# A recurrence in pairs of groups with two MLPs: another order of the work at the end and the start of a pair

## The reference

```python
batch, n_heads, seq, head_dim = (4, 8, 768, 40)
for t in range(S):                       # state: one 40x40 matrix for each of 32 heads
    y[:, :, t] = np.einsum('bhd,bhde->bhe', rt, state)
    Sa = np.einsum('bhde,bhe->bhd', state, at)
    state_decay = state * wt[:, :, None, :] - np.einsum('bhd,bhe->bhde', Sa, bt)
    state = state_decay + np.einsum('bhd,bhe->bhde', vt, kt)
# y as tokens: x (3072, 320)
h = x @ w_in; g = h - np.tanh(h); x = g @ w_out          # d_ff 2048
p = domain_probs / (domain_probs.sum(-1, keepdims=True) + 1e-09)
for e in range(4):                                        # F 1024
    out += p[:, e:e + 1] * (np.maximum(x @ w1[e], 0.0) @ w2[e])
```

## Time and profile before

| | us |
|---|---|
| median of three runs | 1610.46 (1609.79 to 1610.70) |
| the profiled execution, its own time | 1605.92 |
| its span, first to last instruction | 1604.2 |
| PE busy | 1459.2 (91%) |
| DVE busy | 834.7 (52%) |
| ACT busy | 397.8 (25%) |
| POOL busy | 364.9 (23%) |

### The profile page before, as it was taken

How to read it: one execution, slowest core, us unless ns; L and a number is a source line. 1 busy time by engine, 2 the same in 40 slices (tenths; PEclk the granted TensorE clock), 3 DMA queues, 4 the chain that set the end, 5 groups by cost and what they waited for, 6 DMA issues and landing times.

```text
span 1604.2 us, 37826 instructions
## 1 busy us (share of the span) xinstructions
PE 1459.2 (91%) x15888; PEld 1276.4 (80%) x15888; DVE 834.7 (52%) x1460; ACT 397.8 (25%) x814; POOL 364.9 (23%) x310
## 2 busy tenths in 40 slices
PE   2287687999999999999969999999999999999998
PEld 1266566977987887887858888999999999999898
DVE  7978765967967876854213233333333333333333
ACT  1022342333233333333324222111111111111111
POOL 4121453323334332321324301001020202020000
PEclk9988798999999999999989999999999999999999
DMA  7554584056047136121030220101010101000011
GB/s 186 146 138 118 155 204 128 21 142 178 25 121 186 37 95 152 29 65 38 5 106 1 86 70 1 36 0 36 0 36 0 36 0 36 0 0 0 0 49 49
DMA packets 87672, 108.72 MB, mean 68 GB/s; under 512 B 13630, under 2 KB 66686, under 8 KB 87542
## 3 DMA queue, kind: packets, MB, share of 16 engines
q1 hardware_dynamic: 87542, 106.83, 24.8%
HBM read 75.94 MB, written 30.84 MB: 67 GB/s over the span
## 4 chain that ended last, share of the span: by engine, by line
PE 79%; issue 7%; DVE 6%; POOL 3%; POOLq 2%; DMA 1%; ACT 1%; SPq 1%; DVEq 0%; ACTq 0%
PE banks L1543 22%; PE banks L1553 21%; PE banks L887 11%; PE banks L896 10%; PE banks L654 2%; DVE nvmak L1195 2%; PE banks L769 2%; POOLq L1320 1%; PE banks L747 1%; PE banks L734 1%; PE banks L717 1%; PE banks L726 1%; PE banks L773 1%; PE banks L627 1%; POOL wo L1342 1%
## 5 line engine op out<-in xcount | busy, mean ns | idle before, releaser
L1543 PE MATMUL banks<-x2t,u 128*128 (+1 forms) x1536 | 376.7, 392 | 0.0
L1553 PE MATMUL banks<-u,hid 128*128 128x320 f32 x2304 | 362.5, 309 | 0.0
L1553 PEld LDWEIGHTS banks<-u,hid 128*128 128x128 f32 x2304 | 349.8, 188 | 13.0 <-issue 0.9
L1647 DVE SCALAR_TENSOR_TENSOR hid<-banks,hid 128x512 fp32r<-128x512 f32 x192 | 132.8, 692 | 404.4 <-ACT hid L1633 404.4
L1543 PEld LDWEIGHTS banks<-x2t,u 128*128 128x128 f32 x1536 | 282.5, 188 | 52.7
L1633 ACT ACTIVATE hid<-banks 128x512 fp32r<-128x512 f32 x192 | 114.7, 597 | 564.9 <-PE banks L1543 564.9
L887 PE MATMUL banks<-xt,wi 128*128 128x512 f32 x768 | 196.5, 400 | 22.1 <-issue 13.4
L896 PE MATMUL banks<-wo,hid 128*128 128x320 f32 x1152 | 183.0, 309 | 2.0 <-POOL hid L1358 1.6
L887 PEld LDWEIGHTS banks<-xt,wi 128*128 128x128 f32 x768 | 142.4, 191 | 50.5 <-issue 14.7
L896 PEld LDWEIGHTS banks<-wo,hid 128*128 128x128 f32 x1152 | 174.9, 188 | 9.5 <-POOL hid L1358 2.2
L1358 POOL TENSOR_TENSOR hid<-shared,hid 128x512 fp32r<-128x512 f32 x96 | 123.8, 1289 | 222.2 <-ACT hid L1052 222.2
(11 more groups left out here) (117 smaller groups left out, 1550.9 us busy)
## 6 DMA issues: line engine op xcount, KB each, us to landing
scaled_operands<-made SPq DMA_DIRECT2D x79, 192.4 KB
kb<-scaled_operands SPq DMA_DIRECT2D x46, 192.0 KB
made<-kbaw SPq DMA_DIRECT2D x38, 192.0 KB
made<-kbaw SPq DMA_DIRECT2D x41, 144.0 KB
raw<-w SPq DMA_DIRECT2D x8, 640.0 KB, 5.7
lam<-scaled_operands SPq DMA_DIRECT2D x46, 96.8 KB
at<-scaled_operands SPq DMA_DIRECT2D x46, 96.0 KB
raw<-w SPq DMA_DIRECT2D x8, 512.0 KB, 3.9
```

The source lines that it names most:

```text
L1543: mm = pe.matmul(self.p_up[f][:], self.u1[:, par, w, f * 128:(f + 1) * 128], self.xt[:, bass.ds(n, 1), x, :].rearrange("p o t -> p (o t)") ...
L1553: mm = pe.matmul(self.p_dn[t][:, 0:D], self.hid[:, f, h, t * 128:(t + 1) * 128], self.u2[:, par, w, f, :], start=(f == 0 and i == 0), stop ...
L1647: dve.scalar_tensor_tensor(out=ex.hid[:, f, 1, :], in0=ex.p_up[f][:], scalar=0.0, in1=ex.hid[:, f, 0, :].bitcast(F32), op0=ALU.max, op1=AL ...
```

## The change

No instruction is added or taken away; PE, DVE, ACT and POOL get another order, and a few waits move with it. SP's order is the same.

- **End of a pair, PE and ACT.** `turn_answers(p)` comes ahead of `state_by_answers`, `scores_low` behind it, and `natural(p+1, 1)` last. The bank of the transposes is handed over accordingly: `turn_answers` waits for the first natural's copy, the second natural for the turned answers' copy, and `turn_state` and the late diagonals for the second natural's copy.
- **Round 1, PE.** The second diagonal comes behind `right_side_rest`, and `state_by_values` behind `answer` and `result_by_answers`.
- **DVE.** The second half reciprocal of i[1] stood behind `update_state`, ahead of `save_low_rest`. Now it stands in the next pair behind the first two right sides, ahead of that pair's scans. In the last pair of a chunk (p = 3, 7, 11, 15) it stays at the end, behind `save_low_rest`.
- **POOL.** In the first three pairs of a chunk `decay_state` comes between the scaling of i[0] and that of i[1]; before, it came behind both.

```diff
@@ PE: turn_state, turn_answers, natural
-            if p:
-                pe.wait_ge(ut_saved, p)
-                if in_mlp(p - 1):
-                    pe.wait_ge(lt_saved, diagonals_before(p + 1))
-            else:
-                pe.wait_ge(kbn_saved[1], 1)
+            pe.wait_ge(kbn_saved[1], p + 1)
+            if p and in_mlp(p - 1):
+                pe.wait_ge(lt_saved, diagonals_before(p + 1))
...
-                pe.wait_ge(kbn_saved[1], p + 2)
+                pe.wait_ge(kbn_saved[0], p + 2)
...
-            if j:
-                pe.wait_ge(kbn_saved[0], p + 1)
+            if j and p:
+                pe.wait_ge(ut_saved, p)
+            elif j:
+                pe.wait_ge(kbn_saved[0], 1)
@@ PE: pair
             turn_state(p)
-            for i in prepared[1:2]:
-                diagonal(i)
             right_side_rest(p, 0, 1)
             right_side_rest(p, 1, 1)
-            for i in prepared[2:3]:
+            for i in prepared[1:3]:
                 diagonal(i)
-            if p > 2:
-                state_by_values(p)
             answer(p, 0, 1)
             answer(p, 1, 1)
             if p and not after_mlp:
                 result_by_answers(p - 1)
+            if p > 2:
+                state_by_values(p)
...
+            turn_answers(p)
             state_by_answers(p)
             if more:
+                scores_low(p + 1)
                 natural(p + 1, 1)
-                scores_low(p + 1)
-            turn_answers(p)
@@ DVE: pair
+        def second_half_at_end(p):
+            return p > 1 and p % PPC == PPC - 1
...
+            if p > 2 and prepared_in(p - 1) and not second_half_at_end(p - 1):
+                invert_half(prepared_in(p - 1)[1], 1)
             for k in i[:1]:
                 scan(k, 0)
                 scan(k, 1)
...
             update_state(p)
-            if p > 1 and i:
-                invert_half(i[1], 1)
             if p + 1 < NP:
                 save_low_rest(p + 1)
+            if i and second_half_at_end(p):
+                invert_half(i[1], 1)
@@ POOL: pair
-            for i in made_here:
+            first = 1 if p > 1 and p % PPC < PPC - 1 else len(made_here)
+            for i in made_here[:first]:
                 scale(i)
             decay_state(p)
+            for i in made_here[first:]:
+                scale(i)
```

More of the change, by code:

```diff
@@ L599, in diagonal @@
             if i in late_diagonals:
-                pe.wait_ge(ut_saved, (i - FIRST) // 2 + 1)
+                pe.wait_ge(kbn_saved[1], (i - FIRST) // 2 + 2)
             elif i >= FIRST:
@@ L1030, in pair @@
                 save_natural(p + 1, 0)
-                save_natural(p + 1, 1)
+            save_turned_answers(p)
             if p + 1 < NP:
                 save_low(p + 1)
-            save_turned_answers(p)
+                save_natural(p + 1, 1)
             if tokens_turned_in(p) is not None:
```

## The result

| | before | after |
|---|---|---|
| median of the runs | 1610.12 us (4 runs) | 1620.40 us (4 runs, 1618.32 to 1622.97) |
| ratio | | 1.0068, 95% interval 1.0049 to 1.0086 |
| profiled execution, its span | 1605.92, 1604.2 | 1618.32, 1616.6 |

The changed kernel is 0.7% slower: 10.9 us by the ratio, 12.4 by the two profiled executions. The forecast was 1621.7, with 11.2 us of loss.

What follows compares the result with a forecast made beforehand. The prediction took PE as the bound, busy 63.42 of 68.40 us in pairs 8 to 11. Losses of 7.0 + 1.2 + 2.5 + 0.5 = 11.2 us on 1610.46 gave 1621.7 us, range 1612 to 1626.5.

Steps and rivals of the forecast that it cites:

- Part 1: Pair 17: PE's 0.48 us wait before scores_ur goes; it starts at T (pair's start) + 0.89, rest ends T + 3.56.
- Part 2: Round 1: answers wait for right sides behind DVE's longer chain; round 2 at T + 6.56, before T + 6.57.
- the first rival: Same as The ports do not matter: POOL's scaling and DVE's scans pass each other; chance 0.20.
- Part 3: Eight steady pairs: POOL's scaling holds DVE's second scan, round 2 0.87 us later each; 7.0 us (6.0 to 11.2).
- Part 4: SP's queue: the store waits for later scaling, so raw loads that scans need come late; 1.2 us (0 to 3).
- Part 5: Weights' stage, ahead of the first MLP: POOL's chain and DVE's inverse run later; 2.5 us (0.5 to 5.5).
- Part 6: Pairs 21 to 23: wait before scores_ur shrinks, round 1's right sides lie bare for 0.4; 0.17 slower each, 0.5 us.
- The ports do not matter: Steady pairs: POOL's scaling and DVE's scans pass each other; 1615.3 us, or 1612.3 if loads keep up; chance 0.20.
- POOL wins the race: Steady pairs: both scans wait for POOL, 8 x 1.4 = 11.2 us, time 1625.9; chance 0.13.
- Faster: Wait before scores_ur goes, nothing replaces it as right sides are ready in time; gain 5.8 us, 1604.7; chance 0.07.

Runs made afterwards that it cites:

- e9: Changed kernel, but from pair 8 on POOL's two multiplications for the second unit cut to one column each, rest of that scaling left out; ratio to before 1.0024.
- e3: Changed kernel, but from pair 5 on the first unit's scans stand behind round 1's right sides; ratio to the kernel before 1.0061.
- e10: Changed order on all engines in pairs 0 to 7 only, order of before from pair 8 on; ratio to the kernel before 1.0027.
- e7: Order of before in pairs 0 to 7 on all engines, changed order from pair 8 on; ratio to the kernel before 1.0047.
- e1: Changed order on PE and ACT only, DVE and POOL as in the kernel before; ratio to that kernel 1.0013.
- e2: Changed order on DVE and POOL only, PE and ACT as in the kernel before; ratio to that kernel 1.0081.
- e8: Kernel before with one move: state_by_values from ahead of round 1's answers to behind result_by_answers, from pair 3 on; ratio 1.0029.
- e11: Order of before to pair 7; then changed kernel with both units' scans moved later, raw load earlier, result_by_answers covering round 1's answers; ratio to before 0.9976.
- e5: Changed kernel, but from pair 5 on SP issues the second unit's raw load ahead of its late store; ratio to the kernel before 1.0063.

## Why the forecast held, step by step

- **Part 1, the wait that goes: right.** `scores_ur` starts at T + 0.87 (T + 0.89), the rest of round 1 ends at 606.07, T + 3.55 (T + 3.56).
- **Part 2, what is late next: right number, wrong engine.** I had DVE's chain at T + 4.69 and round 2 at T + 6.56. DVE's two undisturbed scans take 0.60 start to start, not the 0.86 of rows 3, which stand beside a POOL instruction themselves. The first of them takes 0.62 there instead of 0.36, and ends 0.28 behind POOL's 104x256 multiplication: these rows, which I had held for the first rival, already were the collision. Without it, in `e9`, the right sides let the answers start at T + 4.17. What holds them without the collision is the diagonal behind POOL's scaling, at T + 4.61 in `e3`, with round 2 at T + 6.50. I had seen that chain end at the same time and treated it as an echo. So without the collision the change would gain nothing either, but because the scaling is released late, and not because DVE has too much in front.
- **Part 3, the collision: right in mechanism and place, somewhat too large.** Scan 1 passes, POOL starts, scan 2 waits and ends 0.29 behind POOL's first instruction (I took 0.28 from rows 5 and 6). The mask starts at T + 3.73; I had 3.88, since I gave POOL 0.2 us of delay by scan 1, and it had none: it starts 0.08 behind the reciprocal's end and takes 1.27, in `e3` too, where no scan is near. Round 2 came 0.75 later, and the end of the pair gave 0.08 back: the clean pair grew by 0.67, not 0.87. Pairs 11 and 15, which end a chunk, keep 0.71 (73.63 us to the next chunk in `e10`, 74.34 in `e7`). So the eight pairs cost 5.4 us, and not 7.0. Pairs behind an MLP, which I had put at 0, start round 2 at T + 8.63 in place of 7.63 and give most of it back: the shortest of them takes 18.36, against 18.19. The order of the race, DVE first, was the same in all steady pairs, as the 0.05 us of rows 3 and 4 said.
- **Part 4, the loads: a little too dear.** 0.6 us for 1.2. SP's store comes at T + 4.31 (T + 4.45), and the scans wait 9.9 us in all, up to 2.1. But right sides that are themselves 0.75 later hide it, except in pairs 13 and 18.
- **Part 5, the weights' stage: too small.** 2.5 us forecast; 3.4 by difference and 4.3 by `e10`, inside my 0.5 to 5.5. From pair 5 to the first MLP the executions with the new order are 1.8 us longer than that of before on average (six of them), those of variants with the old order 0.5 (four): the forecast had 1.2 + 0.3, and the weights of pair 5 start at T + 4.44 (T + 4.5), below. What I missed lies ahead of pair 5, where I had 1.0. Pair 5 starts 2.4 to 4.0 later there with the new order (five of six), and -1.1 to 2.5 with the old. Which of the moves does it isn't settled: from pair 2 to the first MLP `e1` and `e2`, with half of the engines each, take 150.0 and 149.4 us, both more than any execution with the old order.

```profile
203.20 1.27 POOL L1339 TENSOR_TENSOR wi<-spare,wi 128x512 fp32r<-128x512 f32 x1 [0.16 <-issue]
```

- **Part 6, the last three pairs: 0.33 each, not 0.17.** The new order gains 0.16 there (15.66 against the 15.82 of `e8`), nearly the 0.2 forecast, though most of it at the pair's end; the wait ahead of `scores_ur` fell only from 0.41 to 0.38. The lost cover costs 0.49 by `e8`, and I had put 0.4 on it. Timeline of PE in pair 22 of the changed kernel:

```profile
744.39 1.16 PE L744 MATMUL banks<-rt,shared 40*128 40x128 f32 x16 [0.38 <-DVE low L1187]
...
747.44 0.72 PE L654 MATMUL banks<-rhs,tt 128*32 128x160 f32 x4 [0.37 <-DVE rhs L1161]
```

- **The sum.** From pair 8 on 7.5 us (8.7 forecast; pair by pair 5.4 + 0.6 + 1.0 = 7.0), ahead of it 3.4 to 4.3 (2.5), in all 10.9 (11.2). Two terms were too large and two too small. That they cancel to 0.3 us is luck.
- **The rivals.** *The ports do not matter* falls with `e9`. *POOL wins the race* didn't happen in any steady pair. *Faster* failed where its condition said: the answers start at T + 5.20, far behind T + 3.92. `e11` shows that this rival's gain was there to be had once the scans, the load and the cover were moved along.

By the Trainium skill ("SBUF — State Buffer", "Who interferes with whom") a DVE instruction with two inputs in SBUF and one of GpSimd that reads SBUF take turns for whole instructions. Scan 2 agrees: it waited its 1.04 us. So do the mask with one input in PSUM (1.19 to 1.21) and the reciprocal with one input (1.74 beside `tokens_lo` in `e9`, and 1.74 with POOL idle in the changed kernel), which waited nothing. Scan 1 doesn't agree: POOL's multiplication starts 0.20 us before that scan ends and takes its 1.27 as if alone, where by the rule it would have been held.

## What to carry to other kernels

An instruction that is moved out of one wait carries its consumers with it: ask what the engine behind it will start, and which two-input instructions of DVE stand at that moment. Where DVE's work sits between two of PE's steps, count what PE has to do meanwhile; an independent block of PE is worth the wait that it covers, so swap covers, never just delay one. Take an instruction's own time from a place where its neighbour is idle, and compare several executions before a difference of 2 us in one stage is put down to an edit.

## What the chip showed besides

The clock ahead of the first MLP. PE idles there for 8.6 us, the granted clock falls to 0.50, and how soon it comes back differs between executions. Windows of 6 us, first before, then after:

```profile
260.00:266.00 6.00, 2.41 (x6) 1.93 (x7) 0.00 (x0) 0.00 (x0) 3.22 (x3) 0.50 0.25 79
266.00:272.00 6.00, 6.00 (x44) 4.37 (x42) 2.18 (x3) 1.49 (x3) 0.00 (x0) 0.79 0.10 30
272.00:278.00 6.00, 6.00 (x34) 5.32 (x33) 5.48 (x11) 1.58 (x4) 2.60 (x2) 1.00 0.23 62
```

```profile
266.00:272.00 6.00, 3.35 (x8) 2.49 (x8) 0.00 (x0) 0.00 (x0) 2.28 (x3) 0.50 0.14 53
272.00:278.00 6.00, 6.00 (x26) 4.27 (x24) 1.92 (x2) 0.60 (x1) 0.00 (x0) 0.51 0.09 27
278.00:284.00 6.00, 6.00 (x43) 5.27 (x43) 4.81 (x8) 2.23 (x4) 2.58 (x2) 1.00 0.24 62
```

The matmuls began at 263.6 and 268.65. The stretch at 1.2 GHz behind them was some 4 us longer after (by the clock's means, it ended at about 268.5 and at 278), and from the first MLP to pair 8 it took 61.7 us instead of 59.8. The fourteen executions fall into two kinds. In ten the stretch lasts 3 to 5.5 us and the way to pair 8 takes 58.9 to 60.1; in four (after, `e5`, `e8`, `e9`) it lasts 9 to 9.6 us and the way takes 61.7 to 61.9. So 1.9 of the 7.0 us at pair 8 are this stretch. Three of the four have the new order ahead of the MLP, as three of the ten do, and none of the five with the old order is among them; whether the order has a part in it isn't shown.

Stalls of PE for "issue", 0.3 to 1.35 us at a time, come at other places in each execution, and one load of the raw data came so late in `e3` that DVE waited 4.51 us:

```profile
377.76 0.74 DVE L1087 TENSOR_TENSOR_SCAN made<-made 104x128 f32<-104x128 f32 x2 [4.51 <-DMA made<-kbaw]
```

What makes a single load late wasn't tried.
